# Reordering the first loads, and the fourth chunk's decay work, in a fused linear-attention and two-expert kernel

## What is computed

```python
for t in range(S):                                   # attention, per batch and head
    cur = einsum('bhd,bhe->bhde', u * k_t, v_t)
    y[t] = einsum('bhd,bhde->bhe', r_t, state + cur)
    state = w_t[..., None] * state + einsum('bhd,bhe->bhde', k_t, v_t)

h = x @ w_in1                                        # 384 -> 1024
e = exp(h - max(h)); sm = e / (sum(e) + 1e-9)
solu = h * sm
ln = (solu - mean) / sqrt(var + 1e-6) * g_ln
x2 = ln @ w_out1                                     # 1024 -> 384

h2 = x2 @ w_in2                                      # 384 -> 2048
out = maximum(0.01 * h2, h2) @ w_out2                # 2048 -> 384
```

## Time and profile before

| | |
|---|---|
| median of three runs | 785.93 us (785.57 to 787.09) |
| the profiled execution, its own time | 786.64 us |
| its span, first to last instruction | 784.80 us |
| PE busy | 777.4 us, 99% of the span |
| PE weight loads busy | 734.1 us, 94% |
| VectorE (DVE) busy | 520.1 us, 66% |
| ScalarE (ACT) busy | 341.5 us, 44% |
| GpSimd (POOL) busy | 174.5 us, 22% |
| DMA | 45.89 MB, mean 58 GB/s |

### The profile page before, as it was taken

How to read it: one execution, slowest core, us unless ns; L and a number is a source line. 1 busy time by engine, 2 the same in 40 slices (tenths; PEclk the granted TensorE clock), 3 DMA queues, 4 the chain that set the end, 5 groups by cost and what they waited for, 6 DMA issues and landing times.

```text
span 784.8 us, 12142 instructions
## 1 busy us (share of the span) xinstructions
PE 777.4 (99%) x4638; PEld 734.1 (94%) x4638; DVE 520.1 (66%) x1024; ACT 341.5 (44%) x676; POOL 174.5 (22%) x199
## 2 busy tenths in 40 slices
PE   8999999999999999999999999999999999999998
PEld 4789999899999999999999999999999999999998
DVE  7998999966665676657747567485674766543432
ACT  3577654434344354343434443344343444334333
POOL 4632422321222211212212123022120221100000
PEclk9999999999999999999999999999999999999999
DMA  9961022212113022030120210202202111000001
GB/s 277 278 234 41 26 66 66 57 41 66 36 31 96 1 66 60 7 95 13 54 66 1 97 49 18 66 9 88 66 1 66 36 62 31 1 1 30 1 1 35
DMA packets 20065, 45.89 MB, mean 58 GB/s; under 512 B 1968, under 2 KB 14768, under 8 KB 20000
## 3 DMA queue, kind: packets, MB, share of 16 engines
q1 hardware_dynamic: 15952, 37.17, 15.7%
q10 hardware_dynamic: 4048, 7.87, 3.0%
HBM read 40.31 MB, written 4.72 MB: 57 GB/s over the span
## 4 chain that ended last, share of the span: by engine, by line
PE 80%; DVE 1%; issue 0%; ACT 0%; DVEq 0%
PE BANKS L1186 56%; PE MISC L1186 20%; PE BANKS L1365 2%; PE MISC L1210 1%; PE MISC L1203 1%; DVE ki L870 0%; DVE W2L L1018 0%; DVE att L860 0%; DVE A L883 0%; DVE Rraw L1002 0%; DVE RL L1009 0%; DVE X2L L1024 0%; ACT X2H L739 0%; ACT OUT L745 0%; DVE diag L890 0%
## 5 line engine op out<-in xcount | busy, mean ns | idle before, releaser
L1186 PE MATMUL BANKS<-RH,W4H 128*128 128x384 f32 x384 | 135.4, 353 | 0.0
L1186 PE MATMUL BANKS<-X2H,W3H 128*128 128x384 f32 x384 | 130.8, 341 | 0.2 <-DVE X2L L1024 0.2
L1186 PE MATMUL BANKS<-X2L,W3H 128*128 128x384 f32 x384 | 129.3, 337 | 0.0
L1186 PE MATMUL BANKS<-X2H,W3L 128*128 128x384 f32 x384 | 129.2, 336 | 0.0
L1186 PE MATMUL BANKS<-RH,W4L 128*128 128x384 f32 x384 | 129.1, 336 | 0.0
L1186 PE MATMUL BANKS<-RL,W4H 128*128 128x384 f32 x384 | 129.0, 336 | 0.0
L1002 DVE TENSOR_TENSOR Rraw<-BANKS,Rraw 128x384 f32<-128x384 f32 x128 | 70.6, 552 | 87.1 <-ACT Rraw L718 86.1
L718 ACT ACTIVATE Rraw<-BANKS 128x384 f32<-128x384 f32 x128 | 62.6, 489 | 137.2 <-PE BANKS L1186 136.9
L722 ACT ACTIVATE RH<-Rraw 128x384 fp32r<-128x384 f32 x128 | 67.1, 524 | 100.8 <-DVE Rraw L1002 100.8
L870 DVE RECIPROCAL ki<-att 112x128 f32<-112x128 f32 x96 | 89.5, 937 | 0.0
L1009 DVE TENSOR_TENSOR RL<-Rraw,RH 128x384 fp32r<-128x384 f32 x128 | 71.6, 560 | 22.5 <-ACT RH L722 22.5
(11 more groups left out here) (141 smaller groups left out, 1495.7 us busy)
## 6 DMA issues: line engine op xcount, KB each, us to landing
att<-rkw SPq DMA_DIRECT2D x23, 672.0 KB, 4.8
rtok<-r_tok SPq DMA_DIRECT2D x22, 192.0 KB, 2.5
ktok<-k_tok SPq DMA_DIRECT2D x22, 192.0 KB, 2.9
vtok<-v_tok SPq DMA_DIRECT2D x22, 192.0 KB, 3.6
out<-OUT SPq DMA_DIRECT2D x7, 576.0 KB, 4.3
W3raw<-w_in ACTq DMA_DIRECT2D x2, 1536.0 KB, 10.4
W4raw<-w_out ACTq DMA_DIRECT2D x1, 3072.0 KB, 16.6
W1raw<-w_in SPq DMA_DIRECT2D x2, 768.0 KB, 12.3
```

Source lines behind the costliest of these rows:

```text
L1186: return nc.tensor.matmul(dst, lhsT, rhs, start=start, stop=stop, skip_group_check=True)
```

## The change

The loads at the start are put in another order. Chunk 1's decays get a load of their own, right behind chunk 0's. Then come ub and the tokens of chunk 0. Then SyncE waits until chunk 0's r and k have landed before it issues chunk 1's, and waits for ub before it issues the first half of W1. GpSimd does own_token(0, 0, 0) ahead of end_keys(0, 0). decayed_queries and undecayed_keys wait for the load of r and k themselves. On VectorE, own_sums(0, 0) stands ahead of both inverses. The fourth chunk's decay, inverses and what follows from them move behind the third chunk's moments; three of the low parts of W1 take their former place, and the fourth goes behind step f = 1 of the loop. ScalarE's take_range(0, 3) stands behind part_heads(0, 3). VectorE's inverse(0, 4, 0) stands behind take_x2. TensorE makes one product less that nobody reads.

```diff
-LOW_PARTS = {1: ((3, 1),), 2: ((3, 2), (2, 4)), 5: ((3, 3),), 6: ((3, 4), (1, 0)), 7: ((2, 5), (2, 6)), 10: ((3, 5),),
+LOW_PARTS = {1: ((3, 1), (0, 3)), 2: ((3, 2), (2, 4)), 5: ((3, 3),), 6: ((3, 4), (1, 0)), 7: ((2, 5), (2, 6)), 10: ((3, 5),),
...
+            def load_decay(m):
+                sp.dma_start(att[:, m, 2, :, :].rearrange("p a t -> p (a t)"),
+                             rkw[m * PD:(m + 1) * PD, 2 * PAIRS * CH:3 * PAIRS * CH]).then_inc(ld_decay[m], 16)
...
-                if first(b, m) and m == 0:
-                    sp.dma_start(to[:, 2, :, :].rearrange("p a t -> p (a t)"),
-                                 rkw[0:PD, 2 * PAIRS * CH:3 * PAIRS * CH]).then_inc(ld_decay, 16)
+                if first(b, m) and m < 2:
+                    if m == 0:
+                        load_decay(0)
                     both, part = slice(0, 2), slice(0, 2 * PAIRS * CH)
...
             load_T(0, 0)
+            load_decay(1)
+            sp.dma_start(ub[:, :], u.partition_broadcast(CH)).then_inc(ld_u, 16)
+            load_tok(0, 0)
+            sp.wait_ge(ld_T[0], 16)
             load_T(0, 1)
-            load_tok(0, 0)
-            sp.dma_start(ub[:, :], u.partition_broadcast(CH)).then_inc(ld_u, 16)
+            sp.wait_ge(ld_u, 16)
             columns = w_in1.rearrange("(k p) n -> p k n", p=128)
             sp.dma_start(w1[:, :, 0:512], columns[:, :, 0:512]).then_inc(ld_w1a, 16)
...
             def decayed_queries(b, m):
+                if first(b, m):
+                    wait_T(pool, b, m)
...
             decayed_queries(0, 0)
-            end_keys(0, 0)
             pool.wait_ge(ld_u, 16)
             own_token(0, 0, 0)
+            end_keys(0, 0)
             own_token(0, 0, 1)
...
             row_scale(0, 0)
-            decayed_queries(0, 3)
-            decayed_state(0, 3)
             row_scale(0, 1)
             own_token(0, 3, 0)
             row_scale(0, 2)
+            decayed_queries(0, 3)
+            decayed_state(0, 3)
             end_keys(0, 3)
...
             normalise(0, 2)
-            take_range(0, 3)
             take_ln(2)
             part_heads(0, 3)
+            take_range(0, 3)
             high_part(3, 0)
...
             def undecayed_keys(b, m, portion=(0, PAIRS)):
                 a, n = portion
+                if first(b, m):
+                    wait_T(dve, b, m)
...
-            inverse(0, 1, 0)
             own_sums(0, 0)
-            inverse(0, 1, 1)
+            for a in (0, 1):
+                inverse(0, 1, a)
...
             take_state(0, 2)
-            decay(0, 3)
-            for a in (0, 1):
-                inverse(0, 3, a)
+            for g in range(3):
+                low_part(0, g)
             row_max(0, 1)
...
             row_max(0, 2)
-            inverse(0, 3, 2)
             times_exp(0, 2)
             row_stats(0, 2)
             row_moments(0, 2)
-            inverse(0, 3, 3)
+            decay(0, 3)
+            for a in range(PAIRS):
+                inverse(0, 3, a)
             undecayed_keys(0, 3)
             for g in range(2, 4):
                 low_part(2, g)
-            for g in range(4):
-                low_part(0, g)
             low_part(3, 0)
             decay(0, 4)
+            take_x2(0, 0)
             inverse(0, 4, 0)
-            take_x2(0, 0)
...
             first_state(0)
-            unread(1)
             first_transposes(0)
```

More of the change, by code:

```diff
@@ L257, in build @@
         consts, chain = sem("consts"), sem("chain")
-        ld_decay, ld_w1a, filled = sem("ld_decay"), sem("ld_w1a"), sem("filled")
+        ld_decay = [sem("ld_decay0"), sem("ld_decay1")]
+        ld_w1a, filled = sem("ld_w1a"), sem("filled")
         ld_w3a = sem("ld_w3a")
@@ L853, in decay @@
             def decay(b, m):
-                if first(b, m) and m == 0:
-                    dve.wait_ge(ld_decay, 16)
+                if first(b, m) and m < 2:
+                    dve.wait_ge(ld_decay[m], 16)
                 else:
```

## The result

The kernel before ran at a median of 785.97 us in five executions (785.57 to 787.09), the changed kernel at **789.86 us** (787.75, 788.58, 789.86, 790.66, 791.42). The ratio is 1.0039, with an interval of 1.0028 to 1.0050 (it is not the quotient of the two medians, which is 1.0049): slower, and above the upper end of the range. The two sets overlap, and their 13 executions together have a median of 788.8.

The account below looks back on a forecast made before the run. TensorE was taken to hardly ever stop from 17.78 to about 144 us. Terms -1.35 up front, +0.85 at stage 2's start and +0.9 at the expert product made +0.4: 785.93 + 0.4 = 786.3 us, range 784.8 to 788.1.

Parts of the forecast that it names:

- +1.75 from the later part: Losses after the opening: +0.85 us at stage 2's start and +0.9 at chunk 3's expert product.
- 0.85 at stage 2's start: Moved take_range(0,3) puts take_x2 at 65.1; TensorE waits 0.8 us before its first X2H product; +0.85 in the sum.
- 0.9 at the expert product: W1's fourth low part, straight ahead of take_x(0,3), delays XL; TensorE goes on at 78.8; +0.9 us in the sum.
- Price zero: VectorE behind the third chunk's moments: half a microsecond more ahead of low_part(3,0), which waits for ScalarE anyway; no cost.
- The bounds on the expert product: Chunk 3's expert product starts at 78.5 (+0.1) with all the lead kept on VectorE, 79.0 (+0.6) with none.
- s, the shift of 1.35 us: Opening: earlier ub and vtok bring take_y from 16.04 to about 14.7, a gain of 1.35 us.
- Both arrive together: Before take_y: y of chunk 0 ready at 14.8, VectorE's inverses done at 14.67, so take_y runs at about 14.7.
- Taking it out is worth nothing by itself: Filler product ahead of chunk 0's transposes: over before take_y ended, TensorE waited 0.5 us behind it; dropping it gains zero.
- would make it wrong altogether: Closing list, unpriced: a stretch at the lower clock after the dropped filler, or a landing order not following the bytes.
- second rival: Held loads come late: W1's first half lands at 18.2, first expert product 0.4 later than before; 788.1 us; chance 0.13.
- the gain did not survive: First rival, gain survives: take_range or the late low part is hidden; 785.4 or 784.6 us; chance 0.25.
- the last rival: Loads don't do what is meant: vtok at 11.35 or later, no shift up front, later prices stay; 787.5 us; chance 0.12.

Follow-up runs that it names:

- back_only: Kernel before with only the later part changed (old loads and first steps, filler kept): 788.34 us, ratio 1.0024.
- back_hi_early: `back_only` with two high parts of W3 moved on ScalarE from behind take_range(0,3) to ahead of take_ln(2): 788.21 us, ratio 1.0023.
- back_low_early: `back_only` with W1's fourth low part made in the opening, ahead of low_part(3,0): 787.04 us, ratio 1.0012.
- before_no_filler: Kernel before with only the filler product ahead of chunk 0's transposes dropped: 786.35 us, ratio 1.0007.
- front_filler: `front_only` with one filler product where TensorE waits for end_keys: 786.47 us, ratio 1.0005.
- no_fillers: Changed kernel with the two remaining fillers, behind chunk 0's scores, dropped as well: 793.02 us, ratio 1.0081.
- filler_mid: Changed kernel with one filler product ahead of the key transposes, where TensorE waits: 788.55 us, ratio 1.0023.
- all_mended: Changed kernel with a filler where TensorE waits for end_keys, two high parts earlier and W1's fourth low part earlier: 787.17 us, ratio 1.0014.
- keys_filler: Changed kernel with end_keys(0,0) back ahead of own_token(0,0,0) and the filler back in its old place: 787.87 us, ratio 1.0023.
- front_best: `front_only` with GpSimd's old order (end_keys first) and the old filler: 786.92 us, ratio 1.0016.
- filler_back: Changed kernel with the dropped filler put back ahead of the first transposes: 790.98 us, ratio 1.0057.
- no_holds: Changed kernel without the two waits on SyncE's queue, so only the order of the loads is new: 792.78 us, ratio 1.0070.
- keys_first: Changed kernel with GpSimd's end_keys(0,0) put back ahead of own_token(0,0,0), no filler: 788.27 us, ratio 1.0029.
- front_only: Changed kernel with the old order from 37 us on, keeping the new loads, first steps and dropped filler: 787.71 us, ratio 1.0034.

## Why the prediction was wrong

**In short.** The forecast was -1.35 from the front and +1.75 from the later part. The +1.75 was right. The -1.35 was the failed term: 0.9 in the profile, and no gain in the ratio of any form of the front that was run. And the dropped filler, put at nothing, costs 2 to 5 us in some executions.

**The two prices further on were right.** ScalarE's 0.85 at stage 2's start and 0.9 at the expert product were to come to 1.75; the marks of `back_only` give 0.9 and 1.6, and its medians 788.34 - 786.38 = 2.0. take_range stood at 61.18 (60.7 foretold), take_x2 at 65.50 (65.1), XL at 78.60 (78.2), the expert product at 79.20 (78.8): each 0.4 or 0.5 late, about as much as the front's shift fell short. One step of this part was incomplete: "Price zero" for what stands ahead of low_part(3,0), because that "waits for ScalarE anyway". It does, and that wait grew with take_range, which is a second chain to X2L of the same length. A second thing was left out of the sum: GpSimd's end_keys(0,3), started by the later take_range, was done at 63.9, but W4L beside it took 0.3 longer. The sum didn't suffer from either; the repair in `back_hi_early` did. The bounds on the expert product (78.5 to 79.0) should have allowed for the front's: it came 0.2 past them.

**The term that was mis-sized is s, the shift of 1.35 us.** Measured in the profiled executions it is 0.9. The loads were nearly as forecast (vtok 10.3 against 10.2, W1's first half 15.2 against 15.5; ub, 8.4 against 7.6, wasn't the last, and T(0,1) without decays at 5.50 + 6.9 = 12.4 against the 10.5 by which the added waits were called free, was wanted after 14). The step that failed is "Both arrive together". VectorE was through with its inverses at about 14.8 (14.67 foretold) and then waited 0.35 us for TensorE's y, because the chain over end_keys was the longer one: GpSimd started at 10.45 instead of 10.2, end_keys ended at 13.54 instead of 13.35, and hand-offs that the sum left out stand behind it. take_y ran at 15.13 instead of 14.7.

**And 0.9 is itself too much for a typical execution.** The old front started the W1raw product at 17.78 in the profile of before, but at 17.58, 17.13 and 17.00 in three kernels with the same front (`back_hi_early`, `back_low_early`, `back_only`). F follows the landing of ub: 12.3 in the profile of before, then 12.1, 11.7 and 11.3, and with ub at 10.6 and no filler `before_no_filler` has 16.32, the earliest of all profiles here, with the *old* loads. The new front gave 16.88, 16.79 and 17.28, and with a filler in the gap 16.74, 16.82 and 17.84 (vtok landed at 11.3 in that last one). The means of the four and the first three are 17.4 and 17.0: one profiled execution had a late opening, and I took its lateness for something that the change would remove. With the filler in the gap the front is worth nothing by its ratio (`front_filler`, +0.4 us, interval -0.3 to +1.1). The forecast of +0.4 was -1.35 plus 1.75; measured it is about 0.4 plus 2.0, which gives roughly the 2.4 by which the nine executions of the changed kernel at 0.999 or more (median 788.6) stand over the kernel before (786.2 over its 108). The other 1.2 up to the measured 789.86 are not accounted for: five executions are few, one of them was at 0.996, and two, at 1.000, were long for a reason that stays open.

**The filler was the step with the wrong sign.** "Taking it out is worth nothing by itself" asked only what TensorE waits for, not what its clock does when it is idle. In the changed kernel's profile TensorE idled 0.64 us ahead of the key transposes, which is new, and 0.58 ahead of the first expert product, as before, and in 4 of 13 executions time was spent at the lower clock. They took 790.9 to 793.6. Shown: dropping this filler alone from the kernel before gave 3 of 11 at 0.997 or 0.998, where that kernel had 1 of 108 below 0.999; without any of the three fillers the clock always fell (`no_fillers`), with one in the gap it never did (`filler_mid`, `front_filler`, `all_mended`: none of 33 under 0.999), and with one in the old place hardly (`keys_filler` none of 10, `front_best` one of 11, but `filler_back` three of 5 at 0.998), and the profiles of `no_holds`, `no_fillers` and `keys_first` have the slow products where they were lost. The text named this, last, among what "would make it wrong altogether", and gave it no chance and no price: with 2 to 5 us in a third of the executions it belonged among the rivals, and the upper end of the range at about 791. Not shown is a profile of the changed kernel itself at the lower clock; both of its profiles were at 1.000.

**The holds.** The forecast went by the byte count alone, which happened to fit: it gave the two waits no part in the earlier landings and a price only in its second rival. That loads queued behind leave those ahead of them alone was not shown. The one profile without the holds speaks against it, with vtok 1.2 us later (11.5 against 10.3) and W1's first half 1.6 later (16.8 against 15.2) when issued 3.4 earlier, but lies only just outside the scatter of those with them. **The rivals:** the gain did not survive; the held loads were not late (15.2, not 18.2), though that rival's 788.1 is nearest to the measured time; the loads did land as was meant, and yet the last rival's price, a front that gives nothing, came true by another way. **VectorE and GpSimd side by side.** end_keys(0,3), clear of the low parts of W1, took 1.05 us from 62.83, where the earlier trace rows had 3.81 beside four of them; the low parts took 0.95 each there and 0.94 to 0.95 in the changed kernel, clear of it. But it ran into W4L, which took 0.3 longer. That the overlap is the reason for either is inferred; no run shows how.

## What to carry to other kernels

A product that nobody reads isn't free to remove because TensorE waits right behind it: ask what its idle time was before and becomes after, and price a fall of the clock in some executions, not only in the one profiled (in `before_no_filler` some 2 us, in 3 of 11). A gain that is read off one profile's opening should be set against other executions of the same loads before it is spent. Where a step is moved ahead of an engine's dense run, follow every product of that run to the end (W4H as well as X2H), or the repair will move one of two equal chains. Where a short step is moved ahead of a long one, ask whether the engine would have done the long one while it waited for the short one's input, as VectorE did with an inverse here (take_y came 0.6 us earlier for it).

## What the runs showed of the hardware

- In these runs the clock was a draw in each execution where TensorE idled by parts in the opening: it fell in 7 of 7 executions of `no_fillers` and 7 of 7 of `no_holds`, in 4 of 13 of the changed kernel, in 4 of 11 of `keys_first`, in 3 of 11 of `before_no_filler`, in none of 33 with a filler in the gap, and once in 108 of the kernel before. A profile in which it held proves little: that of `front_only` held it with 0.98 us busy from 12 to 14, where that of `no_holds` had 0.98 as well and lost it.
- It didn't take a long gap: in `keys_first` it fell at about 16.8 us, and the longest idle stretch of TensorE in the 8 us before was 0.76.
- It fell late in `no_fillers`, at about 14 us, when TensorE had been busy for 1.8 of the last 2 us. Whoever looks for the cause only in the stretch where the clock is low can miss it.
- Once down (0.50), it stayed so for about 3.4 us in `keys_first`, 7 in `no_fillers` and 10 in `no_holds`, with TensorE busy for most of that time (in `no_holds` for 7.4 of the 8 us from 16 to 24).
- Landings of the same load differed between profiled executions of the same order: ub at 10.6 to 12.3 with the old loads, vtok at 9.6 to 11.3 with the new ones and the holds. The one profile without the holds had vtok at 11.5, ub at 9.0 (7.4 to 8.5 with them) and the half of W1 at 16.8, each later than in any of the other eleven.
- VectorE's W4L took 1.26 or 1.27 us in twelve profiles where end_keys(0,3) ran beside it, and 0.96 in five where it didn't. In those twelve end_keys(0,3) took 1.05; in the five, where it ran beside the low parts of W1, 3.81 to 4.07.
